# mLSTM, gated MLP and mixture of experts in one kernel: a new memory layout for the split v, w_spatial by halves, and w1's loads

## The reference

```
# 1: mLSTM with gates: y[b,t] from q, k, v and the gates (state C, n, m per head, stepped over t)
# 2: gated MLP with spatial mixing
h = relu(x @ w_in)                                   # 320 -> 1024
u, v = h[..., :512], h[..., 512:]
v_n = (v - mean(v)) / sqrt(var(v) + 1e-6)            # over the 512
v_s = einsum('ts,bsd->btd', w_spatial, v_n) + b_spatial[None, :, None]
x = (u * v_s) @ w_out                                # 512 -> 320
# 3: one of 8 experts per token
logits = x @ w_gate;  local = sigmoid(x @ w_local)
e = argmax(logits[b,s]) if s == 0 or local < 0.5 else the expert of token s-1
out[b,s] = softmax(logits)[e] * (relu(x @ w1[e]) @ w2[e])     # 320 -> 1024 -> 320
```

## Time and profile before

| | us |
|---|---|
| median of three runs (lowest, highest) | 393.53 (392.85, 394.63) |
| the profiled execution | 394.44 |
| its span in the trace | 392.7 |
| TensorE busy (2420 products) | 363.7, 93% |
| VectorE busy | 289.0, 74% |
| ScalarE busy | 208.2, 53% |
| GpSimd busy | 188.6, 48% |
| mean granted TensorE clock, share of full | 0.973 |

### The profile page before, as it was taken

How to read it: one execution, slowest core, us unless ns; L and a number is a source line. 1 busy time by engine, 2 the same in 40 slices (tenths; PEclk the granted TensorE clock), 3 DMA queues, 4 the chain that set the end, 5 groups by cost and what they waited for, 6 DMA issues and landing times.

```text
span 392.7 us, 8052 instructions
## 1 busy us (share of the span) xinstructions
PE 363.7 (93%) x2420; PEld 311.1 (79%) x2420; DVE 289.0 (74%) x548; ACT 208.2 (53%) x453; POOL 188.6 (48%) x208
## 2 busy tenths in 40 slices
PE   7969999999999999999998975899999999999952
PEld 3858999999999889999997633488888878888842
DVE  3676887878786987351657883789898998998940
ACT  2774464646552750243112411678877878787820
POOL 3496536363531302303030232677877777777710
PEclk9989999999999999999999996999999999999976
DMA  8997759585840070002922995994322221211100
GB/s 119 192 187 151 143 148 176 138 144 136 150 156 36 5 264 0 22 0 101 340 84 84 329 355 150 299 391 151 118 62 64 79 82 53 69 52 38 39 6 8
DMA packets 71490, 50.27 MB, mean 128 GB/s; under 512 B 52682, under 2 KB 63211, under 8 KB 71452
## 3 DMA queue, kind: packets, MB, share of 16 engines
q1 hardware_dynamic: 67676, 39.49, 38.8%
q0 software_dynamic: 1808, 5.31, 4.5%
q10 hardware_dynamic: 1968, 4.98, 3.9%
HBM read 45.40 MB, written 4.87 MB: 128 GB/s over the span
## 4 chain that ended last, share of the span: by engine, by line
PE 78%; DVE 8%; SPq 5%; DMA 3%; issue 2%; ACT 1%; POOL 1%; DVEq 0%; ACTq 0%; POOLq 0%
PE psum L1871 14%; PE psum L1671 13%; PE psum L1836 11%; PE psum L1551 6%; PE psum L1540 5%; PE psum L1504 4%; PE psum L1848 4%; PE psum L1856 3%; PE psum L1751 3%; PE psum L1494 3%; PE psum L1516 2%; PE psum L1523 2%; DMA arena<-x_rows,arena 2%; SPq L378 2%; PE psum L1817 1%
## 5 line engine op out<-in xcount | busy, mean ns | idle before, releaser
L664 POOL TENSOR_TENSOR late<-w1m,late 128x512 fp32r<-128x512 f32 x47 | 64.8, 1393 | 23.3 <-ACT late L933 22.3
L1402 DVE TENSOR_TENSOR late<-arena,late 128x640 fp32r<-128x640 f32 x60 | 60.5, 1029 | 10.2 <-ACT late L944 4.7
L1871 PE MATMUL psum<-late,xt_high_low 128*128 128x320 f32 x300 | 56.7, 322 | 2.2 <-DVE xt_high_low L1397 1.8
L1671 PE MATMUL psum<-halves 128*128 128x384 f32 x288 | 54.4, 340 | 0.2 <-DVE halves L1157 0.2
L933 ACT ACTIVATE late<-w1m 128x512 fp32r x62 | 38.8, 632 | 27.4 <-PE psum L1836 19.9
L1836 PE MATMUL psum<-late 128*128 128x512 f32 x180 | 51.2, 416 | 2.0 <-DVE late L1392 0.8
L1871 PEld LDWEIGHTS psum<-late,xt_high_low 128*128 128x128 f32 x300 | 47.9, 196 | 2.7 <-DVE xt_high_low L1397 2.1
L1671 PEld LDWEIGHTS psum<-halves 128*128 128x128 f32 x288 | 49.3, 188 | 0.8 <-issue 0.7
L944 ACT ACTIVATE late<-arena 128x640 fp32r x60 | 44.2, 740 | 7.1 <-PE psum L1871 1.9
L1836 PEld LDWEIGHTS psum<-late 128*128 128x128 f32 x180 | 31.9, 193 | 11.4 <-POOL late L664 4.0
L1281 DVE TENSOR_TENSOR early<-psum,arena 128x384 f32<-128x384 f32 x16 | 8.9, 556 | 29.0 <-PE psum L1671 28.9
(11 more groups left out here) (271 smaller groups left out, 730.4 us busy)
## 6 DMA issues: line engine op xcount, KB each, us to landing
arena<-in_moe_w_dram SPq DMA_DIRECT2D x8, 1280.0 KB, 9.6
w1m<-in_moe_w_dram SPq DMA_DIRECT2D x8, 1024.0 KB, 8.0
early<-m_rows SPq DMA_DIRECT2D x10, 512.0 KB, 4.8
arena<-in_moe_w_dram SPq DMA_DIRECT2D x38, 128.0 KB, 2.9
arena<-in_moe_w_spatial_dram ACTq DMA_DIRECT2D x6, 384.0 KB, 4.3
x_rows<-early SPq DMA_DIRECT2D x12, 192.0 KB, 2.2
arena<-in_q_dram SPq DMA_DIRECT2D x12, 160.0 KB, 3.9
arena<-in_k_dram SPq DMA_DIRECT2D x12, 160.0 KB, 5.0
```

The lines of the kernel that those rows point to most:

```text
L664: g.tensor_tensor(w1l[k % 2], w1m[:, ds(e * 2 * FF + k % 2 * FF + k // 2 * 512, 512)], w1h[k % 2].bitcast(fp32), ALU.subtract).then_inc(m_ ...
L1402: V.tensor_tensor(w2l[:, i * QW:(i + 1) * QW], w2s[:, ds(e * NFT * DM + i * QW, QW)], w2h[:, i * QW:(i + 1) * QW].bitcast(fp32), ALU.subtr ...
L1671: last = T.matmul(PS[n % 4][:, 0:HALF], v_[:, v_at:v_at + P], w_[:, w_at:w_at + HALF], start=s_ == 0 and i == 0, stop=s_ == NC - 1 and i == 2)
L1871: last = T.matmul(PS[5][:, 0:DM], h_[m // 4][:, m % 4 * P:(m % 4 + 1) * P], w_[:, m * DM:(m + 1) * DM], start=m == 0 and h_ is hsh and w_ ...
```

## The change

Memory: `arena` gives up 4096 words a partition. q's, k's rows and their transposes move into `heads`, in front of `halves`; the same words are vn_front, which later has vnh's six pieces and vnl's first two. vnl's pieces 2 to 5 lie over w_in's low half. w_spatial's halves are laid out by halves of the positions: half 0 in front of w_in's halves, half 1 behind. w1m lies over all of it from the front, and w1t behind w1m (w1_rest). So w1 of 0 and 1 lie over v, w1 of 2 to 4 over half 0 of w_spatial and w_in, w1 of 5 over w_in.

w_spatial is turned in ten pieces, five for each half (4, 4, 4, 4 and 2 blocks), with other banks. ACT's norm_high(0) loses its wait and comes ahead of pieces 7 to 9; DVE's norm_low(0) comes ahead of ws_low(7 to 9) and waits for u_ps 12 before piece 2. TensorE's six idle products and the wait ahead of them are gone, and spatial(n) waits only for the pieces of its own half.

SP's order: w1 of 5 behind w2 of 6 and 7 (and u_ps 12); w1 of 2, 3, 4 behind w2 of 2, when 12 of the 16 spatial outputs are done; w1 of 0 and 1 behind x rows 7 and 8 as before; w2 of 3 directly behind x rows 11, and then the releases of experts 0 to 2. After routing: tail 0, the wait for the gathers, tails 1 to 3, w2 of 4, tails 4 to 6, w2 of 5, w1 of 6 and 7.

```diff
         SHARED = 2 * NFT * DM + FF // 2 + 4 * P + 4 * 512
-        ARENA = WORDS - SHARED - 2 * XT2 - E * 2 * FF
+        FRONT = E // 2 * FF
+        ARENA = WORDS - SHARED - 2 * XT2 - E * 2 * FF - FRONT
         W2_AT = ARENA - E * NFT * DM
-        W1R_AT = W2_AT - E // 2 * FF
         arena = ctx.enter_context(nc.sbuf_tensor("arena", [P, ARENA], fp32))
...
         xth, xtl = [xt_high_low[:, i * XT2:(i + 1) * XT2].rearrange("p (k b t) -> p k b t", k=KD, b=B) for i in range(2)]
-        with nc.sbuf_tensor("halves", [P, E * 2 * FF], fp32r) as halves_tensor:
-            halves = halves_tensor[:, :]
+        with nc.sbuf_tensor("heads", [P, FRONT], fp32) as heads_tensor:
+            heads = heads_tensor[:, :]
+        with nc.sbuf_tensor("halves", [P, FRONT + E * 2 * FF], fp32r) as halves_tensor:
+            vn_front, halves = halves_tensor[:, 0:FRONT], halves_tensor[:, FRONT:]
         w1m = ctx.enter_context(nc.sbuf_tensor("w1m", [P, E * 2 * FF], fp32))[:, :]
+        w1_rest = ctx.enter_context(nc.sbuf_tensor("w1_rest", [P, FRONT], fp32))[:, :]
         psum = ctx.enter_context(nc.psum_tensor("psum", [P, 4096], fp32))
...
-        s1 = region(CONST, W1R_AT)
+        s1 = region(CONST, W2_AT)
...
-        s3 = region(CONST, W1R_AT)
+        s3 = region(CONST, W2_AT)
...
-        xs = [s3(XW), arena[:, W2_AT - XW:W2_AT]]
+        xs = [s3(XW), w1_rest[:, FRONT - XW:FRONT]]
...
-        w1t = [arena[:, W1R_AT + i * 512:W1R_AT + (i + 1) * 512] for i in range(NB3)]
-        assert NB3 * 512 + XW <= W2_AT - W1R_AT and NT3 - NB3 <= NSURE
+        w1t = [w1_rest[:, i * 512:(i + 1) * 512] for i in range(NB3)]
+        assert NB3 * 512 + XW <= FRONT and NT3 - NB3 <= NSURE
         w2s = arena[:, W2_AT:ARENA]
-        ov1 = region(W1R_AT, W2_AT)
+        ov1 = region(0, FRONT, heads)
         qb = [ov1(H * DP) for _ in range(B)]
...
-        wih, wil = [halves[:, i * KD * F1:(i + 1) * KD * F1].rearrange("p (k n) -> p k n", k=KD) for i in range(2)]
+        WSN = NC * HALF
+        WI_AT, WS_AT, BEHIND = 2 * WSN, (0, 2 * WSN + 2 * KD * F1), 4 * WSN + 2 * KD * F1
+        wih, wil = [halves[:, WI_AT + i * KD * F1:WI_AT + (i + 1) * KD * F1].rearrange("p (k n) -> p k n", k=KD)
+                    for i in range(2)]
         assert REM == P - REM
-        vnh, vnl = [halves[:, i * NC * FH:(i + 1) * NC * FH] for i in range(2)]
-        WSH = 2 * KD * F1
-        wsh, wsl = [halves[:, WSH + i * NC * S:WSH + (i + 1) * NC * S] for i in range(2)]
+        FRONT_LOW = FRONT // FH - NC
+        vnh = [vn_front[:, c * FH:(c + 1) * FH] for c in range(NC)]
+        vnl = [vn_front[:, (NC + c) * FH:(NC + c + 1) * FH] if c < FRONT_LOW else
+               halves[:, WS_AT[1] - (NC - c) * FH:WS_AT[1] - (NC - c - 1) * FH] for c in range(NC)]
+        wsh, wsl = [[halves[:, at + i * WSN:at + (i + 1) * WSN] for at in WS_AT] for i in range(2)]
         GW = NDT * P
-        behind = halves[:, WSH + 2 * NC * S:WSH + 2 * NC * S + GW]
+        behind = halves[:, BEHIND:BEHIND + GW]
         gth, gtl = [[t.rearrange("p (k s) -> p k s", k=NDT) for t in two] for two in (
             [xt_high_low[:, i * GW:(i + 1) * GW] for i in range(2)], [xt_high_low[:, 2 * GW:3 * GW], behind])]
-        assert NC * FH <= KD * F1 and WSH + 2 * NC * S + GW <= E * 2 * FF and 3 * GW <= 2 * XT2
+        assert (NC - FRONT_LOW) * FH <= KD * F1 and BEHIND + GW <= E * 2 * FF and 3 * GW <= 2 * XT2
+        W1_HALF = range((FRONT + 2 * FF - 1) // (2 * FF), (FRONT + WI_AT + KD * F1) // (2 * FF))
+        W1_IN = W1_HALF.stop
+        assert FRONT + WI_AT <= W1_IN * 2 * FF and (W1_IN + 1) * 2 * FF <= FRONT + WS_AT[1] - (NC - FRONT_LOW) * FH
...
-        NWS, WS2, WS3 = NC * NC // 4, 2, 7
-        WS_BANK = (0, 3, 1, 4, 0, 2, 3, 1, 0)
+        NWS, WS2, WS3 = 10, 2, 7
+        WS_BANK = (0, 3, 1, 4, 0, 2, 3, 4, 2, 3)
+        HT = NC // 2
+
+        def piece(n):
+
+            half, k = divmod(n, NWS // 2)
+            return half, 4 * k, min(4, NC * HT - 4 * k)
+
+        def said_ws(half, s_):
+
+            return half * NWS // 2 + (HT * (s_ + 1) - 1) // 4 + 1
+
+        def piece_of(t, n):
+            half, at, blocks = piece(n)
+            return t[half][:, at * P:(at + blocks) * P]
...
                 load_w2(e)
+            sp.wait_ge(u_ps, 2 * NC)
+            load_w1(W1_IN)
             for n in range(NTT):
...
                     load_w2(2)
+                    sp.wait_ge(sp_ps, B * 2 * NDT - NDT)
+                    for e in W1_HALF:
+                        load_w1(e)
                 if n == NC + 1:
                     sp.wait_ge(sp_ps, B * 2 * NDT)
-                if NC < n <= NC + EARLY:
-                    load_w1(n - NC - 1)
-                if n == NC + EARLY + 1:
-                    load_w1(EARLY)
+                    load_w1(0)
+                if n == NC + 2:
+                    load_w1(1)
+            sp.wait_ge(wo_ps, NTT)
+            load_w2(EARLY)
             for e in range(EARLY):
...
                 sp.sem_inc(w12_ok, 1)
-            load_w1(EARLY + 1)
-            sp.wait_ge(wo_ps, NTT)
-            load_w2(EARLY)
             sp.wait_ge(r_te, TE_ALL)
-            for j in range(2):
-                load_w1_tail(j)
+            load_w1_tail(0)
             for i in range(2):
                 sp.wait_ge(d_xs[i], 16)
-            for j in range(2, 4):
+            for j in range(1, 4):
                 load_w1_tail(j)
             for e in range(EARLY + 1, E):
-                if e > EARLY + 1:
+                if e > W1_IN:
                     load_w1(e)
...
                 act.wait_ge(ws_ps, n + 1)
-                A.activation(wsh[:, n * 512:(n + 1) * 512], PS[WS_BANK[n]], ACT.Copy).then_inc(ws_sb, 1)
+                A.activation(piece_of(wsh, n), PS[WS_BANK[n]][:, 0:piece(n)[2] * P], ACT.Copy).then_inc(ws_sb, 1)
...
                     act.wait_ge(vn_ok, b * NC + c + 1)
-                    A.activation(vnh[:, c * FH:(c + 1) * FH], vr[b][:, c * FH:(c + 1) * FH],
-                                 ACT.Copy).then_inc(vn_hi, 1)
+                    A.activation(vnh[c], vr[b][:, c * FH:(c + 1) * FH], ACT.Copy).then_inc(vn_hi, 1)
...
             A.activation(vr[1][:, (NC - 1) * FH:], PS[6], ACT.Relu).then_inc(v_sb[1], 1)
+            norm_high(0)
             for n in range(WS3, NWS):
                 turned_ws(n)
-            act.wait_ge(u_ps, 2 * NC)
-            norm_high(0)
             projected_both(NC - 1)
...
                 dve.wait_ge(ws_sb, n + 1)
-                V.tensor_tensor(wsl[:, n * 512:(n + 1) * 512], PS[WS_BANK[n]],
-                                wsh[:, n * 512:(n + 1) * 512].bitcast(fp32), ALU.subtract).then_inc(ws_lo, 1)
+                V.tensor_tensor(piece_of(wsl, n), PS[WS_BANK[n]][:, 0:piece(n)[2] * P],
+                                piece_of(wsh, n).bitcast(fp32), ALU.subtract).then_inc(ws_lo, 1)
...
                     dve.wait_ge(vn_hi, b * NC + c + 1)
-                    V.tensor_tensor(vnl[:, c * FH:(c + 1) * FH], vr[b][:, c * FH:(c + 1) * FH],
-                                    vnh[:, c * FH:(c + 1) * FH].bitcast(fp32), ALU.subtract).then_inc(vn_lo, 1)
+                    if b == 0 and c == FRONT_LOW:
+                        dve.wait_ge(u_ps, 2 * NC)
+                    V.tensor_tensor(vnl[c], vr[b][:, c * FH:(c + 1) * FH], vnh[c].bitcast(fp32),
+                                    ALU.subtract).then_inc(vn_lo, 1)
...
             norm(0)
+            norm_low(0)
             for n_ in range(WS3, NWS):
                 ws_low(n_)
-            norm_low(0)
             statistics(1, NC - 1)
...
                     pe.wait_ge(ws_lo, max(i for i in range(n) if WS_BANK[i] == WS_BANK[n]) + 1)
-                for m in range(4):
-                    s_, t_ = divmod(4 * n + m, NC)
+                half, at, blocks = piece(n)
+                for m in range(blocks):
+                    s_, t_ = divmod(at + m, HT)
+                    t_ += half * HT
                     last = T.transpose(PS[WS_BANK[n]][:, m * P:(m + 1) * P],
...
             project_both(NC - 1)
-            pe.wait_ge(ws_lo, max(i for i in range(NWS) if WS_BANK[i] == 4) + 1)
-            warm(6, unit, 4)
-
...
                 for s_ in range(NC):
-                    if n == 0:
-                        pe.wait_ge(ws_lo, (NC * (s_ + 1) - 1) // 4 + 1)
+                    if n in (0, NDT):
+                        pe.wait_ge(ws_lo, said_ws(half, s_))
                     if half == 0 and dt == 0:
                         pe.wait_ge(vn_hi, b * NC + s_ + 1)
-                        pe.wait_ge(vn_lo, b * NC + s_ + 1)
-                    v_at, w_at = s_ * FH + dt * P, s_ * S + half * HALF
                     for i, (v_, w_) in enumerate(((vnh, wsh), (vnh, wsl), (vnl, wsh))):
-                        last = T.matmul(PS[n % 4][:, 0:HALF], v_[:, v_at:v_at + P], w_[:, w_at:w_at + HALF],
+                        if half == 0 and dt == 0 and v_ is vnl:
+                            pe.wait_ge(vn_lo, b * NC + s_ + 1)
```

(2 more changed lines are left out.)

## The result

The changed kernel takes 392.17 us (median of 13 runs, 390.34 to 394.67), the kernel before 394.72 in the 13 runs beside them: a ratio of 0.9942, 95% interval 0.9914 to 0.9971, so 2.3 us faster, give or take 1.1. (The ratios are those on record for the two sets of runs; they are not the quotients of the medians, here 0.9935.) I had forecast 387.0, 384.4 to 390.3. The direction was right, the size was not: 5.2 us are missing. The profiled execution took 392.87, its span is 391.1.

The account below looks back on a forecast made before the run. TensorE was taken as the bound, busy 363.7 of 392.7 us, with gains only where the chain leaves it or its clock is low. A 1.65 + B 3.5 + C 1.5 = 6.65 us gave 387.0, range 384.4 to 390.3.

Parts of the forecast that it names:

- B: End of routing: moved weight loads let the first gather land sooner, so TensorE inverts the weights 3.5 us earlier.
- C: First expert tile: TensorE's clock stays full behind the routing pause, so the second tile follows sooner, 1.5 us.
- A: Start of spatial mixing: ACT splits v while project_both still runs, so the first spatial product comes 1.65 us earlier.
- R2: Rival at the end of routing: the clock falls in the sparse 3 us from 234.2; 388.4 us, 14%.
- R1: Rival at the end of routing: first gather takes 7.7 us even without loads beside it, clock falls; 391.2 us, 10%.
- R3: Rival at the start of spatial mixing: DVE paces spatial(0), the early split gains near 0; 388.5 us, 6%.
- R4: Rival in spatial mixing: new places of v and w_spatial slow each of 288 products, at 30 ns 395.5 us, 4%.
- R5: Rival near the end: shifted work meets the clock otherwise, last tile regains 2.1 us of half-clock time; 384.8 us, 9%.

Follow-up runs that it names:

- before_again: The kernel before, unedited, run once more on another chip for a second trace: 395.88 us.
- before_third: The kernel before, unchanged, run in the third batch for one more trace of the first phase: 393.92 us.
- before_filled: The kernel before with 45 idle TensorE products instead of 20 behind the first inversion in routing: 392.9 us, ratio 0.9956.
- lows_later: The changed kernel with GpSimd's first two w1 lows made to wait for DVE's one-hot of the weights: 387.66 us, ratio 0.9826.
- clock_kept: The changed kernel with 11 more idle products between the first transpose of x and the inversion of the weights: 389.98 us, ratio 0.9865.
- lows_filled: lows_later with 27 idle products instead of 20 ahead of the first turned x: 390.09 us, ratio 0.9864.
- lows_and_clock: lows_later with five idle products between the first transpose of x and the second inversion: 388.6 us, ratio 0.9856.

## Why the prediction was wrong

The step that failed is B's 3.5 us: it let GpSimd's lows hold back one DVE instruction, the one-hot, and took one trace's 240.83 for the kernel before; the copy of 12 elements is held back instead, and B measures 1.8. C's 1.5 us failed with it: the clock did not stay. The three traces of each unchanged kernel, cut at the same events (us; the mean of after less the mean of before in the fourth column):

| stretch | before | after | difference | forecast |
|---|---|---|---|---|
| start to the last project_both | 135.60, 135.59, 137.76 | 137.30, 139.69, 136.61 | +1.55 | 0 |
| to the first spatial product (A) | 5.61, 5.62, 5.62 | 3.91, 3.91, 3.91 | -1.71 | -1.65 |
| to the first inversion | 87.94, 89.08, 87.94 | 87.87, 87.86, 88.99 | -0.08 | 0 |
| to the first tile (B) | 12.15, 11.31, 10.33 | 9.56, 9.56, 9.31 | -1.79 | -3.5 |
| to the second tile (C) | 7.05, 7.62, 6.60 | 7.67, 6.88, 6.95 | +0.08 | -1.5 |
| to the last product | 137.17, 137.75, 136.75 | 137.64, 136.63, 137.35 | -0.02 | 0 |

From project_both on the change is worth 3.5 us by these traces, where I had summed 6.65; 3.5 us would be a ratio of 0.9911, just under the first interval (0.9914 to 0.9971) and within the second (0.9841 to 0.9937). With the first row it is 2.0 us in all, 0.995.

**Part A was right**, in mechanism, in size and in its slack: two low halves, the wait for project_both, four more, and no later stall. The 36 blocks in ten pieces cost nothing to see.

**Part B, the term that was mis-sized.** The steps came one by one: the last x row landed in 2.1 us, the gather started at 231.38 (I said 231.5) and was quick, GpSimd's lows ended at 236.4 (236.5), and DVE was what came last. Two numbers in it failed. First, what the lock holds back. I priced DVE's one-hot as the blocked instruction, since the trace of before showed it so, at 3.73 us. But there the gather and the lows had started 0.7 us late, behind an x row write that took 7.8; with the gather released by DVE the lows come that much sooner and hit the copy of 12 elements, as they do in the kernel before in before_again, before_third and before_filled too. lows_later shows the cause: with the lows behind it the copy takes 0.19 us. Four more instructions, the one-hot the last, then come behind the lows: 236.44 to 238.0, 1.6 us, instead of the 0.74 that I took. Second, what B was measured from. The 240.83 came from one trace, whose second inversion is 11.47 behind the first (it starts at 240.62; 240.83 is where the chain of waits passes to it); two later traces of the same kernel show 10.63 and 9.65. Its late gather, 0.65 us of my 3.5, was of that one trace too. My own lower bound of 2.9 lay above what the mean shows, 1.8, because it bounded the new side alone and took the old one as fixed.

That DVE waits out GpSimd's work was in the forecast. The Trainium skill (SBUF — State Buffer, "SBUF: two separate sides") gives the shared port pair, between a GpSimd instruction and a VectorE one in a 2-port mode or with two SBUF inputs, to whichever starts first, and the other is blocked in full. The trace agrees on the block, with a copy of 0.19 us turned into 3.20, and it is longer than one low of 1.25: the copy came through only behind both. It doesn't bear out who goes first: by the recorded starts the copy is 0.65 us ahead of the lows, and the one-hot of the trace of before 0.49 (GpSimd's recorded starts are rough).

**Part C failed**, and was rival R2. From 234.1, the end of the 20 idle products, to 238.06 TensorE had one group of three transposes, and the clock fell near 236.9; it fell in all three traces of the change. I had inferred from before, 1.00 through 234 to 238 with 0.18 us of work, that three sparse microseconds were safe. What that row shows is when the clock fell in one trace with its own dense work ahead, not that a like pause keeps it. clock_kept shows 1.4 us to be real where the clock is held and the halves of w1 are ready.

**The base.** 387.0 was counted from the median of three runs, 393.53. The kernel before took 394.72 to 394.94 in four sets of 13 to 23 runs, the first of which holds those three. Of the 5.2 us by which I missed, 1.2 are this and 3.1 are the parts (B 1.7 and C 1.6 short, A and the stretches that I had at 0 behind it 0.2 over). The remaining 0.9 may be of the first phase, or chance: the change's two medians are 0.7 apart (392.17 and 391.49).

R1, a gather slow by itself, is excluded (3.5 to 4.0 us where the loads are out of its way, 5.0 and 6.6 to 7.7 beside them), and with it the time that its 391.2 stood for; that number is nearer to the truth than mine by chance. The Trainium skill (DMA: Bandwidth & Descriptors, "Queues, rings and completion order") has the DMA engines take turns between queues; if that spares a small gather, it spares it only in part here. R3 and R4 are excluded by the rows above. R5's clock at the end falls in every trace, for 6.8 us in thirteen of them and 10.2 in lows_filled, and no gain of R5's kind is seen.

## What to carry to other kernels

When an edit removes the last of several waits, walk down the next engine's whole instruction list to the product it feeds, and ask of each instruction on it whether the other engine's work now meets it: a lock hits the first one in its way, however small, and all behind it pay. Two causes can hide each other (here the slow gather and the lows: 1.8 us at this place for the gather alone, no change of the time for the lows alone, 3.9 at this place for both); test them together. Count a gain from the mean of several traces of the old kernel, since single ones differ by 2 us in one wait, and before a pause in TensorE is taken as safe for its clock, or filled, ask what else would then pace the same stretch.

## What the runs showed of the hardware

- A VectorE copy of 128x12 elements takes 0.19 us alone and 3.20 when GpSimd's two subtractions of 128x512 (2.50 together) are in its way; the small float32 instructions just ahead of it, not beside the lows, ran at 0.17 to 0.26. It isn't the copy alone: in lows_later a float32 tensor_tensor of 128x19 beside the moved lows takes 1.11 us, where it takes 0.18 in the changed kernel.
- One indirect gather of 128 rows took 3.5 to 4.0 us in the new order of loads (eight traces), 5.0 beside the old order in the new layout (one), and 6.6 to 7.7 in the old layout and order (five).
- The granted clock held with 25 or 7 idle products more ahead of the pause (before_filled, lows_filled) and with 11 or 5 in it (clock_kept, lows_and_clock), and fell in all ten other traces, between 236.1 and 240.3.
- The first 136 us of one and the same kernel differ by up to 3.1 us between executions (136.61 to 139.69), and the stretch from the first spatial product to the first inversion by 1.1: in six of the 14 traces, of both kernels, the clock is at half for 3.4 us from between 214 and 217, and they take 88.9 to 89.3 us; the eight others take 87.9. In before_again, one of the six, the clock shows 0.83 from 210 to 220.
